# A fused attention, spectral mixer and gated-MLP kernel on one core: one right tap ahead of another in the last step, the last two normalised units written by VectorE, and their transposes in chunks 2 and 4

## What is computed

```python
def attention(q, k, v, S1, S2):            # (4, 4, 1088, 32), S1 and S2 (8, 32)
    q_p, k_p = phi(q), phi(k)              # phi: outer product of two sketches, 64 features
    kv = einsum('bhsf,bhsd->bhfd', k_p, v)
    z = sum(k_p, axis=2)
    return einsum('bhsf,bhfd->bhsd', q_p, kv) / (einsum('bhsf,bhf->bhs', q_p, z)[..., None] + 1e-6)

def mixer(x, w_ch1, w_ch2):                # x (4, 1088, 128): the four heads side by side
    u = x + real(fft(fft(x, axis=1), axis=2))
    un = (u - mean(u)) / sqrt(var(u) + 1e-6)
    return u + maximum(un @ w_ch1, 0) @ w_ch2          # 128 -> 512 -> 128

def gated(x, w_in, conv_w, w_out):
    h = maximum(x @ w_in, 0)               # 128 -> 1024
    conv = conv_w[0] * h[s - 1] + conv_w[1] * h[s] + conv_w[2] * h[s + 1]
    return (h * sigmoid(conv)) @ w_out     # 1024 -> 128
```

## Time and profile before

| what | value |
|---|---|
| median of 3 runs | 253.71 us (253.62, 253.71, 286.54) |
| the profiled execution | 254.01 us, span of its instructions 252.2 us |
| granted TensorE clock | 1.00 in all the slices |
| TensorE busy | 243.8 us (97% of the span) |
| VectorE busy | 213.2 us (85%) |
| ScalarE busy | 172.8 us (68%) |
| GpSimd busy | 53.4 us (21%) |

### The profile page before, as it was taken

One profiled execution on the slowest core, in us unless ns is written; L12 is line 12 of the kernel. 1 busy time (PEld: TensorE's weight loads), 2 busy tenths in 40 slices (PEclk: granted clock), 3 DMA queues, 4 the chain that ended last, 5 costly groups with the idle time before them and its releaser, 6 DMA issues.

```text
span 252.2 us, 4440 instructions
## 1 busy us (share of the span) xinstructions
PE 243.8 (97%) x1558; PEld 215.6 (85%) x1558; DVE 213.2 (85%) x400; ACT 172.8 (68%) x342; POOL 53.4 (21%) x123
## 2 busy tenths in 40 slices
PE   8999999999999999997999999999999999999975
PEld 6999999999989998996978788998789889887743
DVE  0757888899998697897979899978969999989972
ACT  2342634332576556778899898999958989988832
POOL 0000000000614541665401332121411311221100
PEclk9999999999999999999999999999999999999999
DMA  6968830200000020000004789396986637997402
GB/s 235 342 245 309 351 99 3 65 36 0 3 0 0 4 83 4 0 3 3 0 0 88 194 251 224 128 177 180 273 213 135 166 105 226 262 195 194 95 3 88
DMA packets 9094, 31.41 MB, mean 125 GB/s; under 512 B 1264, under 2 KB 2032, under 8 KB 9072
## 3 DMA queue, kind: packets, MB, share of 16 engines
q0 software_dynamic: 4752, 18.35, 30.5%
q1 hardware_dynamic: 4176, 12.74, 13.8%
q10 hardware_dynamic: 144, 0.03, 0.1%
HBM read 10.54 MB, written 2.23 MB: 51 GB/s over the span
## 4 chain that ended last, share of the span: by engine, by line
PE 48%; DVE 4%; ACT 3%; issue 1%; ACTq 0%
PE ps L702 12%; PE ps L611 10%; PE ps L613 10%; PE ps L612 10%; PE ps L651 5%; DVE attic L1192 1%; ACT arena L824 1%; DVE attic L1185 1%; ACT attic L910 1%; PE ps L642 1%; DVE attic L1170 1%; PE ps L621 0%; DVE x_room L1084 0%; DVE arena L1091 0%; DVE x2lo L1118 0%
## 5 line engine op out<-in xcount | busy, mean ns | idle before, releaser
L910 ACT ACTIVATE attic<-attic,base 128x1088 f32<-128x1088 f32 x32 | 37.8, 1204 | 5.6 <-DVE attic L1185 5.6
L702 PE MATMUL ps<-attic,wout 128*128 128x364 f32 (+1 forms) x120 | 39.1, 469 | 1.4 <-DVE attic L1192 1.4
L611 PE MATMUL ps<-x2hi,wlo 128*128 128x364 f32 x96 | 37.3, 389 | 0.8 <-ACT arena L838 0.5
L702 PEld LDWEIGHTS ps<-attic,wout 128*128 128x128 f32 x120 | 22.5, 189 | 14.5 <-issue 2.1
L613 PE MATMUL ps<-x2hi,whi 128*128 128x364 f32 x96 | 31.6, 329 | 0.0
L612 PE MATMUL ps<-x2lo,whi 128*128 128x364 f32 x96 | 31.5, 328 | 0.0
L611 PEld LDWEIGHTS ps<-x2hi,wlo 128*128 128x128 f32 x96 | 18.1, 188 | 5.1 <-ACT folded_room L895 1.2
L456 POOL TENSOR_SCALAR arena<-arena 109x4 f32<-109x4 f32 x10 | 2.0, 197 | 88.8 <-DVE arena L1097 88.7
L895 ACT ACTIVATE x_room<-ps 128x364 f32<-128x364 f32 x42 | 18.2, 478 | 3.5 <-PE ps L613 3.2
L1185 DVE SCALAR_TENSOR_TENSOR attic<-x_room,ratio,attic 128x1088 f32<-128x1088 f32 x14 | 18.7, 1346 | 2.1 <-DMA attic<-x_room 2.0
L612 PEld LDWEIGHTS ps<-x2lo,whi 128*128 128x128 f32 x96 | 18.1, 188 | 2.5 <-issue 1.1
(11 more groups left out here) (129 smaller groups left out, 616.3 us busy)
## 6 DMA issues: line engine op xcount, KB each, us to landing
gate_hi<-attic POOLq DMA_DIRECT2D x12, 544.0 KB, 3.6
attic<-folded_room POOLq DMA_DIRECT2D x9, 544.0 KB, 5.2
attic<-x_room POOLq DMA_DIRECT2D x8, 544.0 KB, 5.5
attic<-v_d SPq DMA_DIRECT2D x4, 594.0 KB, 3.8
attic<-qT_d SPq DMA_DIRECT2D x3, 545.0 KB, 6.8
attic<-kT_d SPq DMA_DIRECT2D x3, 544.5 KB, 5.6
attic<-arena POOLq DMA_DIRECT2D x3, 544.0 KB, 5.7
out_d<-arena SPq DMA_DIRECT2D x3, 544.0 KB, 4.7
```

The source lines that it names most:

```text
L611: pe.matmul(out, lo, rhi, start=first, stop=False)
L702: pe.matmul(ps[:, OUT_BANK + t, 0:z - a], wout[:, c, :], gate(i)[:, a:z], start=(c == 0), stop=(c == C2 - 1)).then_inc(wout_done, 1)
L910: act.activation(gate(i), gate(i), ACT.Sigmoid, scale=base[:, i % C2:i % C2 + 1]).then_inc(gate_ready, 1)
```

## The change

Three things change.

1. In step 31 the right tap of chunk 30 stands ahead of chunk 31's on VectorE. `RIGHT_ORDER`, from which the sigmoids take the count they wait for, follows.
2. The rows of places 8 and 9 are written by VectorE (`late_rows`, four `tensor_scalar` of 109x128 for each) in place of ScalarE's four ACTIVATEs. Place 8's stand in slot 21 behind `normed_low(7)`, place 9's behind the right tap of chunk 0. A semaphore of their own, `un_late`, tells TensorE.
3. The transposes of place 8 move from behind `hidden(0)` to behind `hidden(2)`, those of place 9 from behind `hidden(3)` to behind `hidden(4)`. `normed_high` and `normed_low` of both move along.

```diff
-RING, LAST_TURNS = 6, {0: 8, 3: 9}
+RING, LAST_TURNS = 6, {2: 8, 4: 9}
+VECTOR_ROWS = (8, 9)
...
         def rights(step):
-            return [i for i in (step, step - ADDED_LATE) if 0 <= i < NI and i + late(i) == step]
+            both = (step - ADDED_LATE, step) if step == NI - 1 else (step, step - ADDED_LATE)
+            return [i for i in both if 0 <= i < NI and i + late(i) == step]
...
             def normed_transposes(r):
 
-                pe.wait_ge(un_ready, 2 * BP * (r + 1))
+                if r in VECTOR_ROWS:
+                    pe.wait_ge(un_late, 2 * BP * (VECTOR_ROWS.index(r) + 1))
+                else:
+                    pe.wait_ge(un_ready, 2 * BP * (r + 1))
...
-                if n in ROWS_AT:
+                if n in ROWS_AT and ROWS_AT[n] not in VECTOR_ROWS:
                     normed_rows(ROWS_AT[n])
...
             relu(0)
-            normed_high(LAST_TURNS[0])
...
                     relu(i + 1)
-                    if i == 0:
-                        normed_rows(NR - 1)
...
+            def late_rows(r):
+                dve.wait_ge(rstd_ready, r + 1)
+                dve.wait_ge(ut_done, r - 1)
+                for m, u in enumerate(normalised(TURN_ORDER[r])):
+                    dve.tensor_scalar(un[:, r % 2, m, :], u, rstd[:, r % 3, m:m + 1], shift[:, r % 3, m:m + 1],
+                                      ALU.mult, ALU.add).then_inc(un_late, 1)
...
+                if n in ROWS_AT and ROWS_AT[n] in VECTOR_ROWS:
+                    late_rows(ROWS_AT[n])
...
                 if step == 0:
-                    normed_low(LAST_TURNS[0])
+                    late_rows(NR - 1)
```

More of the change, by code:

```diff
@@ L233, in build @@
             sem(n) for n in ("stats_ready", "mv_ready", "pow_step", "rstd_ready", "un_ready", "half_set"))
-        ut_done, unhi_ready, unlo_ready = (sem(n) for n in ("ut_done", "unhi_ready", "unlo_ready"))
+        un_late, ut_done, unhi_ready, unlo_ready = (sem(n) for n in ("un_late", "ut_done", "unhi_ready", "unlo_ready"))
         w1_done, h1hi_ready, h1lo_ready, w2_done = (
```

## The result

The changed kernel takes 252.19 us, the one before 253.80 us in the same comparison: ratio 0.9936, 95% interval 0.9921 to 0.9951. That is 1.6 us or 0.6% less, clear of 1 by its own interval and far inside 2%. The prediction's "about 2%" for what can be told from no change was much too wide. The forecast was 252.0 us, 1.74 us less.

What follows compares the result with a forecast made beforehand. TensorE hardly ever stops and was taken as the bound, with few stops in the first chunks, at chunk 9 and in the tail; 1.24 + 0.5 = 1.74 us off 254.01, less 0.30, gives 252.0 us, range 251.0 to 253.4.

Steps and rivals of the forecast that it cites:

- Part 1, the right taps: Tail, step 31: chunk 30's tap first starts its sigmoid 1.26 us earlier and gives 1.24 us, bounds 0 to 1.37.
- The bound at chunk 9: First chunks: VectorE's taps delay sigmoids and chunk 8's ReLU, so TensorE gains no more than VectorE, 0.5 not 0.6 us.
- The four stops: TensorE's stops in the first chunks: 0.64 + 0.57 + 0.25 + 0.23 = 1.7 us, the most the front could give.
- A row on VectorE: Price of one TENSOR_SCALAR of 109x128 in late_rows: 0.18 us, 0.7 for four, between bounds 0.09 and 0.48.
- Place 8's rows: VectorE, early: the four rows run from 118.36 to 119.1 us in idle time, before chunk 0's ReLU ends; free.
- The wait for GpSimd: VectorE, before place 9's rows, behind chunk 0's right tap: a new wait of 0.9 us for GpSimd's last step.
- Chunk 0: TensorE's stop at 118.34 goes as rows leave ScalarE, 0.64 us; place 8's moved transposes give 0.4 us only until chunk 2.
- Chunks 3, 4 and 6: TensorE: wait before chunk 4 stays, ends 0.75 us earlier; uncovered transposes leave 0.35; 0.6 us ahead at chunk 6.
- The rule that was weighed: Shared port of VectorE and GpSimd: the pow would delay place 8's rows, leaving VectorE 0.2 us and giving 252.3.
- The slower rival: VectorE late in step 0, a row costing 0.6 us: chunk 9 starts 2.1 us late, 254.6 us; chance 0.06.
- the two that gave nothing: Rivals: front gives nothing, 252.5 us, chance 0.18; tail gives nothing, 253.2 us, chance 0.04.
- the full relief of ScalarE: Rival, first chunks: all four TensorE stops vanish as ScalarE loses 3.3 us of work, 251.2 us; chance 0.12.

Runs made afterwards that it cites:

- e1: The kernel before with only the two right taps of step 31 swapped; 252.44 us, ratio 0.9964 to the kernel before.
- e4: The changed kernel with place 9's four rows written a second time by VectorE, into a buffer nothing reads then; ratio 0.9969 to the kernel before.
- e5: The changed kernel with place 9's rows and place 8's low part behind chunk 1's right tap on VectorE; ratio 0.9927 to the kernel before.
- e6: The changed kernel with VectorE's split of w_out moved from step 3 to behind the right taps of step 5; ratio 0.9922 to the kernel before.
- e9: The changed kernel with the edits of e5 and e6 together; ratio 0.9933 to the kernel before.
- e3: The changed kernel with transposes, high and low parts of places 8 and 9 in their old places, rows still on VectorE; ratio 0.9961 to the kernel before.
- e7: The changed kernel with the rows of places 8 and 9 on ScalarE again, transposes still moved and taps swapped; ratio 0.9975 to the kernel before.
- e12: The changed kernel itself measured once more, nothing altered; 252.34 us, ratio 0.9959 to the kernel before.

## Why the prediction was right, and where it wasn't

**Part 1, the right taps: right.** Forecast 1.24 us, measured 1.26 in the changed kernel and 1.26 alone (e1). All its steps hold: no wait for the DMA, the sigmoid 1.26 us earlier, room behind chunk 29, nothing late in chunk 31.

**The bound at chunk 9: right.** "What VectorE does in the first steps reaches TensorE here" was read from two waits. e4 puts work there and pays for it at chunk 9; e5 and e6 take work out of the way in two places and gain, and e9 shows that it is one stop. TensorE was 0.69 us ahead at chunk 6 (19.46 in place of 20.15; forecast 0.6) and had 0.39 left at chunk 9. What the prediction missed is that VectorE sets the pace at chunk 7 already, where 0.39 are left as well (22.36 in place of 22.75). ScalarE's list in the changed kernel, the sigmoid ahead of the ReLU of chunk 6:

```profile
135.56 1.21 ACT L915 ACTIVATE attic<-attic,base 128x1088 f32<-128x1088 f32 x1 [0.18 <-DVE attic L1196]
```

The four stops that the prediction adds up to 1.7 us have 0.23 for the one at chunk 9, without a row. TensorE's timeline in the kernel before, the six projections ahead of chunk 9:

```profile
144.41 1.99 PE L702 MATMUL ps<-attic,wout 128*128 128x364 f32 x6
```

Chunk 9 follows at 146.36, 1.95 us later, where six such projections take 1.55 in e6. So this stop was 0.40 us. Neither slip changes the forecast, which VectorE's 0.5 us bounds.

**A row on VectorE: too cheap.** This is the mis-sized term. I took 0.18 us and 0.7 for four; it is 0.26 from row to row and 1.11 for four. One instruction takes 343 ns against 784 for eight and a half times the columns, so most of it doesn't grow with the columns. The nearest row, a TENSOR_TENSOR of the same shape at 0.225 us, should have been kept and not lowered for the missing input. Place 8's rows were free all the same: they end at 119.02 and chunk 0's ReLU at 119.05. The wait for GpSimd was 0.65 us rather than 0.9: the taps began about 0.15 us later than counted (4.35 us behind place 7's transposes; I had 119.4 - 115.19 = 4.2), and GpSimd ended 0.14 us earlier (7.70 for 7.84). In sum VectorE is 0.38 us ahead, forecast 0.5.

**Chunk 0: incomplete.** I gave the 0.64 us to the rows' leaving ScalarE and called the move of place 8's transposes neutral ("afterwards not"). e3 refutes that. In the old place TensorE reaches the transposes before VectorE has written the rows, with the same loss. e7 shows the other half: the move without the rows costs 0.85 us. Only both together gain 0.4. For the kernel as changed the sum came out the same, because its list has both; that much was luck. I had looked for what a moved wait costs in its new place, not in the old one.

**Chunks 3, 4 and 6: right.** The stop before chunk 4 is still there and ends 0.70 us earlier (13.15 in place of 13.85, forecast 0.75). The transposes behind chunk 4 are uncovered: chunk 5 is only 0.31 us ahead (16.52 in place of 16.83), forecast 0.35.

**The rule that was weighed.** VectorE's rows of place 8 started at 117.91, just behind GpSimd's `pow` at 117.86. They took 1.11 us, and the second group, which met no GpSimd instruction, 1.12. So VectorE wasn't kept waiting, and the 252.3 that I worked out by that rule found no support. In the other direction the rows agree with it again: GpSimd's steps at 119.36 and 120.66 took 1.21 and 1.30 us beside the two taps, and 0.20 when VectorE was idle. The rule, that whichever of the two engines issues first keeps the shared ports for its whole instruction, is in the Trainium skill, "SBUF — State Buffer", section "Who interferes with whom". Why the `pow` doesn't hold VectorE up stays open; no run here shows whether these rows use the shared ports at all, or whether the `pow` keeps them for all of its 1.08 us.

**The sum.** 1.26 + 0.39 = 1.65 us by the distances (1.74 in e12) against a forecast of 1.74. The ratio's 1.6 is as close partly by luck, since e12's says 1.0. The slower rival and the two that gave nothing fell; the full relief of ScalarE did too, since the stop before chunk 4 remained.

## What to carry to other kernels

When work goes from one engine to another, look at who reads its result and when: the reader's place in its own list may have to move with it, and either edit alone can be worth nothing or less. A stop that is removed pays only up to the next place where another list sets the pace, so follow the changed list to the next wait that it ends before the gain is booked. An instruction that heads a short chain to the last work of a kernel belongs ahead of its equal on the same engine, if what it reads is there by then; here that gain was the same 1.26 us whatever happened in front.

## What I had not expected

- A TENSOR_SCALAR of 109x128 takes VectorE 343 ns, more than the TENSOR_TENSOR of the same shape with its 287, though it reads one tensor less. It does take two numbers per partition besides; what they cost was not measured.
- The same instructions up to place 7's transposes took between 114.32 and 115.30 us in the profiles that distances are given for, a spread as wide as most of the differences looked for here. Where it arises I didn't follow; distances from a common instruction got round it.
- Behind the exchanged wait, e3's chunks start as in the kernel before to about 0.05 us (13.89 for 13.85 by distance at chunk 4, and 31.21 for 31.17 at chunk 9), although other instructions ran on two engines.
